# Mixing weights, first matrices and first read back on ScalarE's queue, and two late tiles behind the first forward transforms

## What is computed

```python
X = np.fft.rfft(x, axis=1)
Yr = Xr @ w_r - Xi @ w_i + b_r
Yi = Xr @ w_i + Xi @ w_r + b_i
Y = soft_threshold(Yr, 0.01) + 1j * soft_threshold(Yi, 0.01)
y = np.fft.irfft(Y, n=3008, axis=1)            # (6016, 256) as tokens
h = y @ moe_w_in                                # 256 -> 2048
g = maximum(h, 0) + alpha * minimum(h, 0)
z = g @ moe_w_out                               # 2048 -> 256
h2 = z @ moe2_w_in
g2 = where(h2 >= 1, h2, where(h2 <= -1, 0, (h2 + 1) ** 2 / 4))
out = g2 @ moe2_w_out
```

## Time and profile before

| | us |
|---|---|
| median of 3 runs | 1197.14 |
| lowest and highest | 1196.10, 1198.14 |
| the profiled execution | 1194.89 |
| its span | 1193.1 |
| TensorE busy | 1173.4 (98%) |
| VectorE busy | 886.8 (74%) |
| ScalarE busy | 850.2 (71%) |
| GpSimd busy | 691.8 (58%) |

### The profile page before, as it was taken

The page is one execution under the profiler, slowest core; times in us unless marked ns, Lnnn a source line. Parts: engine busy times, 40 slices in busy tenths (PEclk is TensorE's granted clock), DMA queues, the critical chain, the costliest instruction groups (busy, mean ns, idle before and its releaser), DMA issues.

```text
span 1193.1 us, 21060 instructions
## 1 busy us (share of the span) xinstructions
PE 1173.4 (98%) x6948; PEld 1135.1 (95%) x6948; DVE 886.8 (74%) x1686; ACT 850.2 (71%) x1874; POOL 691.8 (58%) x724
## 2 busy tenths in 40 slices
PE   8999999999999999999999999999999999999997
PEld 3899889999999999999999999999999999999997
DVE  4777677777777777777778787778778787878765
ACT  2335557777777777777767788888878787878775
POOL 3006546666575766766556566665657575757553
PEclk9999999999999999999999999999999999999999
DMA  9777620211112101212005500101010101010001
GB/s 307 247 251 238 189 66 1 94 40 54 41 49 72 67 27 41 85 37 67 19 1 177 190 23 2 26 1 27 1 27 1 27 1 24 4 19 9 13 15 27
DMA packets 64125, 77.75 MB, mean 65 GB/s; under 512 B 31216, under 2 KB 43632, under 8 KB 64016
## 3 DMA queue, kind: packets, MB, share of 16 engines
q1 hardware_dynamic: 60532, 69.92, 19.0%
q10 hardware_dynamic: 3484, 6.48, 1.6%
HBM read 46.10 MB, written 30.28 MB: 64 GB/s over the span
## 4 chain that ended last, share of the span: by engine, by line
PE 93%; POOL 3%; ACT 1%; DVE 1%; issue 1%; DMA 1%; SPq 0%; POOLq 0%; DVEq 0%; ACTq 0%
PE bank L1153 80%; PE bank L1120 6%; PE bank L1139 2%; PE bank L1094 2%; PE bank L1130 2%; PE bank L1105 2%; POOL g_lo L515 2%; DMA x_sb<-x 1%; POOL prep_raw L541 0%; POOL xc_lo L490 0%; PE bank L1078 0%; ACT g_hi L762 0%; ACT prep_hi L785 0%; SPq L325 0%; DVE y_sum L856 0%
## 5 line engine op out<-in xcount | busy, mean ns | idle before, releaser
L515 POOL TENSOR_TENSOR g_lo<-g_sb,g_hi 128x376 fp32r<-128x376 f32 x510 | 505.1, 1001 | 374.2 <-ACT g_hi L762 373.7
L1153 PE MATMUL bank<-g_hi,w_out_hi 128*128 128x376 f32 x1024 | 345.1, 337 | 0.9 <-POOL g_lo L515 0.4
L1153 PE MATMUL bank<-g_lo,w_out_hi 128*128 128x376 f32 x1024 | 342.0, 334 | 0.0
L1153 PE MATMUL bank<-g_hi,w_out_lo 128*128 128x376 f32 x1024 | 341.8, 334 | 0.0
L1153 PE MATMUL bank<-xc_hi,w_in_hi 128*128 128x376 f32 x896 | 302.3, 337 | 0.6 <-DVE partial L921 0.2
L1153 PE MATMUL bank<-xc_hi,w_in_lo 128*128 128x376 f32 x896 | 300.4, 335 | 0.0
L1153 PE MATMUL bank<-xc_lo,w_in_hi 128*128 128x376 f32 x896 | 298.5, 333 | 0.0
L762 ACT ACTIVATE g_hi<-g_sb 128x376 fp32r<-128x376 f32 x512 | 261.0, 510 | 44.1 <-DVE g_sb L958 28.5
L1153 PEld LDWEIGHTS bank<-g_hi,w_out_hi 128*128 128x128 f32 x1024 | 192.3, 188 | 8.8 <-POOL g_lo L515 7.6
L1153 PEld LDWEIGHTS bank<-g_lo,w_out_hi 128*128 128x128 f32 x1024 | 192.4, 188 | 0.0
L1153 PEld LDWEIGHTS bank<-g_hi,w_out_lo 128*128 128x128 f32 x1024 | 192.3, 188 | 0.0
(11 more groups left out here) (82 smaller groups left out, 1534.3 us busy)
## 6 DMA issues: line engine op xcount, KB each, us to landing
gc<-group_consts SPq DMA_DIRECT2D x24, 256.0 KB, 4.3
zt<-slots_scratch SPq DMA_DIRECT2D x24, 256.0 KB, 4.2
inverse_scratch<-v_sb SPq DMA_DIRECT2D x24, 256.0 KB, 2.8
ut<-inverse_scratch SPq DMA_DIRECT2D x16, 384.0 KB, 4.8
slots_scratch<-a_sb ACTq DMA_DIRECT2D x15, 384.0 KB, 4.2
x_sb<-x SPq DMA_DIRECT2D x16, 256.0 KB, 4.0
prep_raw<-wpack SPq DMA_DIRECT2D x16, 256.0 KB, 2.6
out<-yt SPq DMA_DIRECT2D x120, 32.0 KB, 1.6
```

What stands on the lines that cost most here:

```text
L515: pool.tensor_tensor(g_lo[kind][:, :], g_sb[n % 3][:, :], g_hi[kind][:, :].bitcast(f32), ALU.subtract)\
L1153: done = pe.matmul(out_ap, w, g, start=first and n == 0, stop=last_one and n == 2, skip_group_check=unchecked)
```

## The change

- `FIRST_TILES` goes from 12 to 11. The late tiles are now 11 to 15, behind `forward` of the steps 0, 1, 4, 8 and 12. Tile 10 is loaded by SyncE with the early ones, ahead of the store of tile 7.
- `wm_raw` and `gc[0]` are issued by ScalarE, right behind its store of tile 7. `zt[0]` is issued by ScalarE behind its copy of tile 9 and a wait for the nine stores; `wm_hi` and, on VectorE, `wm_lo` follow there, ahead of the copies of tile 10.
- SyncE, behind the store of tile 7, issues the tiles 11 and 12 and the bias, and only then waits for the stores, for the pairs 1 and 2.
- `FULL_TILES` goes from 2 to 1: tile 1 is filled by VectorE, a fifth fill, and comes in two transfers.

```diff
-FIRST_TILES = TILES_PER_BATCH + 4
-LATE_TILES = {1: FIRST_TILES, 4: FIRST_TILES + 1, 8: FIRST_TILES + 2, 12: FIRST_TILES + 3}
-LATE_LOADS = {4: FIRST_TILES + 2, 6: FIRST_TILES + 3}
+FIRST_TILES = TILES_PER_BATCH + 3
+LATE_TILES = {0: FIRST_TILES, 1: FIRST_TILES + 1, 4: FIRST_TILES + 2, 8: FIRST_TILES + 3, 12: FIRST_TILES + 4}
+LATE_LOADS = {4: FIRST_TILES + 3, 6: FIRST_TILES + 4}
-FULL_TILES = 2
+FULL_TILES = 1
@@ SyncE
-            for t in range(1, TILES_PER_BATCH + 2):
+            for t in range(1, FIRST_TILES):
                 load_x(t)
             t = TILES_PER_BATCH - 1
             sp.wait_ge(a_right, t + 1)
             sp.dma_start(az_rows[0, 0:ROWS_PAD, t * TILE_COLS + HALF_COLS:(t + 1) * TILE_COLS],
                          a_tile(t)[:, HALF_COLS:]).then_inc(a_stored[0], 16)
-            load_x(TILES_PER_BATCH + 2)
-            load_x(TILES_PER_BATCH + 3)
-            load_matrices(0)
-            sp.wait_ge(a_stored[0], 16 * (TILES_PER_BATCH + 1))
-            load_values(0)
-            sp.dma_start(wm_raw[:, :], wmix).then_inc(wm_in, 16)
             load_x(FIRST_TILES)
+            load_x(FIRST_TILES + 1)
             sp.dma_start(bias_sb[:, :], bias).then_inc(bias_in, 16)
+            sp.wait_ge(a_stored[0], 16 * (TILES_PER_BATCH + 1))
             for p in range(1, SLOTS):
                 load_values(p)
                 load_matrices(p)
-            load_x(FIRST_TILES + 1)
+            load_x(FIRST_TILES + 2)
@@ ScalarE, in the loop over the first tiles
-            act.wait_ge(wm_in, 16)
-            act.activation(wm_hi[:, :], wm_raw[:, :], ACT.Copy).then_inc(wm_hi_ready, 1)
+                if t == TILES_PER_BATCH - 1:
+                    act.dma_start(wm_raw[:, :], wmix).then_inc(wm_in, 16)
+                    act.dma_start(gc[0][:, :], group_consts[0, :, :]).then_inc(gc_in[0], 16)
+                if t == TILES_PER_BATCH + 1:
+                    act.wait_ge(a_stored[0], 16 * (TILES_PER_BATCH + 1))
+                    act.dma_start(zt[0][:, :, :], az_pairs[0, :, :, :]).then_inc(zt_in[0], 16)
+                    act.wait_ge(wm_in, 16)
+                    act.activation(wm_hi[:, :], wm_raw[:, :], ACT.Copy).then_inc(wm_hi_ready, 1)
@@ VectorE, in the loop over the first tiles
-            dve.wait_ge(wm_hi_ready, 1)
-            dve.tensor_tensor(wm_lo[:, :], wm_raw[:, :], wm_hi[:, :].bitcast(f32), ALU.subtract)\
-               .then_inc(wm_lo_ready, 1)
+                if t == TILES_PER_BATCH + 1:
+                    dve.wait_ge(wm_hi_ready, 1)
+                    dve.tensor_tensor(wm_lo[:, :], wm_raw[:, :], wm_hi[:, :].bitcast(f32), ALU.subtract)\
+                       .then_inc(wm_lo_ready, 1)
```

More of the change, by code:

```diff
@@ L365, in _ @@
                          a_tile(t)[:, HALF_COLS:]).then_inc(a_stored[0], 16)
-            load_x(TILES_PER_BATCH + 2)
-            load_x(TILES_PER_BATCH + 3)
-            load_matrices(0)
+            load_x(FIRST_TILES)
+            load_x(FIRST_TILES + 1)
+            sp.dma_start(bias_sb[:, :], bias).then_inc(bias_in, 16)
             sp.wait_ge(a_stored[0], 16 * (TILES_PER_BATCH + 1))
-            load_values(0)
-            sp.dma_start(wm_raw[:, :], wmix).then_inc(wm_in, 16)
-            load_x(FIRST_TILES)
-            sp.dma_start(bias_sb[:, :], bias).then_inc(bias_in, 16)
             for p in range(1, SLOTS):
```

## The result

The changed kernel took 1204.31 us (median of 6 runs, 1200.22 to 1206.23), the kernel before 1197.14 on the same chip (6 runs, 1196.10 to 1198.16). The ratio is 1.0053, 95% interval 1.0039 to 1.0068: slower by about 6 to 7 us, where 3.5 was forecast. The median lies 0.7 us above the upper end of the stated range, 1203.6. The profiled execution took 1204.87 us with a span of 1203.1, 10.0 more than the span of before.

A forecast was written before the change was run, and what follows sets the result against it. TensorE, busy 98% of the span, was taken as the bound, so delay before mix(0) counts in full: +1.3 us (landing of zt[0]) + 2.2 (clock) = +3.5, 1198.4 profiled, 1200.6 us with the 2.25 median offset; range 1195.2 to 1203.6.

The forecast's parts named there:

- What bounds the kernel: Whole kernel: TensorE, busy 98% of the span; what happens before the first mixing product moves everything behind it one for one.
- The order on TensorE: From zt[0]'s landing to mix(0): forward(0), tile 11, forward(1), tile 12 take 4.3 us, against 4.24 before.
- Z: Time at which zt[0] has landed: 30.22 us before, forecast 31.5, ends 30.1 and 33.1; break-even 30.2.
- The landing of zt[0]: Read back ahead of mix(0): loaded queues bring it at 31.5 in place of 30.22, 1.3 us later.
- The stores lose what it takes: Queues in 20 to 22 us: tile 10's 0.39 MB takes bytes from the stores, less 0.13 MB tile 1 no longer carries.
- Tile 1 in two parts: Start of the kernel: tile 1 is down at about 6.5 us, cost nothing, at worst 1 us late.
- the queue argument of the prediction: From 22.2 us on, 1.45 MB up to zt[0] at 0.18 MB/us takes 8.1 us, plus 1.2: landing at 31.5.
- The copies behind the weights: Copies of tile 10 behind the weights' splitting, needed by tile 11: cost nothing, at most about 1 us.
- The clock: After 6.6 us idle behind tile 10, forward(0) and tile 11 run at 1.2 GHz: +2.2 us, bounds 0 and 2.6.
- A: Rival, start of the kernel: zt[0] meets a short queue, lands at 27.8, mix(0) at 32.1; 1194.8 us if clock holds; chance 0.17.
- B: Rival: landing 30.2 with fallen clock (+2.2) or 31.5 with held clock (+1.3); about 1198.9 us; chance 0.30.
- D: Rival: worse sharing, short rows of zt[0] and matrices lose turns; landing 33.1, clock 2.6, +5.5, 1202.6 us; chance 0.15.

The follow-up runs named there:

- e3: The changed kernel with five added products on zeros, results unused, ahead of forward(0); 1201.50 us, ratio 1.0028 to the kernel before.
- j2: The kernel before with only the order moved: tile 11 behind forward(0), wm_hi and wm_lo behind its copies; 1198.80 us, ratio 1.0006.
- j4: The kernel before with weights, first matrices and zt[0] issued by ScalarE, tiles 10 to 12 behind the last store, TensorE order kept; 1198.70 us, ratio 1.0008.
- h1: The kernel before with two added products, results unused, ahead of the fourth token product group; 1196.34 us, ratio 0.9988.
- f2: The changed kernel with tile 1 whole, tile 10 behind tile 7's store, weights and first matrices back on SyncE; ScalarE issues zt[0] alone; 1201.07 us, ratio 1.0025.
- j5: The kernel before with only zt[0] moved, issued by ScalarE behind its copy of tile 9 into an empty queue; 1198.35 us, ratio 1.0004.

## Why the prediction was right in direction and short in size

The forecast was +3.5 us, and it came out at +7.2 in the medians, beyond the upper end of the range (1203.6) by 0.7 us. The direction and the two mechanisms held; one term was mis-sized by 3 us.

- **What bounds the kernel.** Right. All of mix(0)'s delay reached the end; the first product of the layers is later by 9.84 us (167.13 against 157.29) and the end by 10.0.
- **The order on TensorE.** The path Z + 4.3 is right: 4.32 us in e3 at the full clock. That the order in itself costs nothing holds only with Z fixed and the clock held; the profile of j2 shows the cover that it takes away.
- **The landing of zt[0], forecast +1.3, measured +4.35.** This is the term that failed. "The stores lose what it takes" (tile 10) was right as to bytes (0.42 MB in place of 0.74 in 20 to 22), but the step that failed is the issue of zt[0]. The working let it leave near 25 and had the bytes ahead of it in its queue decide; it left at 29.12, because the last store landed that late. I moved only bytes, not instructions: tile 10's two issues also stand ahead of the last store in SyncE's own queue, and they took 1.60 and 1.31 us in place of 0.6. The last store left at 22.56, after a copy done at 21.39, and landed at 29.1 where the working implied about 25. The issue of the last store at 20.48 was carried over from the trace of before unexamined, though that trace has slow issues where both queues are loaded:

```profile
14.27 1.38 SPq L326 DMA_DIRECT2D x_sb<-x  x1
```

  The instructions are the smaller part all the same (1.14 us, and 0.94 by the later copy); most is the store's own landing, 3.0 us slower in the loaded queues. e2, with tile 10 behind the store, has Z at 32.80.
- **Tile 1 in two parts, forecast nothing, at worst 1 us.** Failed as well: "the idle stretch behind tile 10 covers it too, unless it delays the stores" named the condition, and it was met. 0.66 MB fewer by 12 us, waits for the tiles 7 to 10, and 2.2 us at Z in the profile of e1. With tile 1 whole, e1 has Z = 32.37, 2.15 us later than before; in that kernel the queue argument of the prediction (31.5, at most 33.1) would have held.
- **The copies behind the weights.** Nothing, as said: wm_lo and tile 10's copies were done at 32.5, before Z.
- **The clock, forecast +2.2, measured +1.94** in the profile (1.86 by e3). Right, though the idle stretch was 4.74 us, not 6.6, since the tiles ahead of it were late too. That no gap in the trace of before is long enough to test the clock was wrong: its wait of 2.43 us ahead of the fourth token group is such a gap, and behind it the clock fell in nine of twelve profiles.
- **Behind mix(0), forecast nothing.** The profile shows 3.7 us there, which would count as a miss by the prediction's own test. The 0.66 us up to the first token group lies within what `ut` differs by from profile to profile, and the fall near 150 us is found in before as well, so neither is shown to be a cost of the change. The profile-to-median offset of 2.25 us that the prediction added has, by the table above, much to do with this fall.
- **The rivals.** A needed Z below 30.2 and is out. B needs one of its terms missing; both were there. D had the right signs, "the sharing is worse", with Z = 33.1; the measured Z lies 1.5 us beyond it, and by another cause than the short rows that it named.

## What to carry to other kernels

When a transfer is moved ahead of another in one engine's queue, count its issue instructions under load as well as its bytes: of the 2.1 us by which the store behind it left later 1.1 were such instructions, and it landed 3 us more slowly. A transfer that "costs nothing" at the start may still starve the queues there, so look at the bytes moved by the time of the first contention, not only at who waits for the tile. And before two profiled spans are subtracted, see whether the clock fell in one of them at a wait that both have: here that was 2.9 of 10.0 us. One profile of each kernel also hides how far landings scatter: with the same transfers zt[0] left between 27.5 and 30.4.

## What the runs showed of the hardware that was not expected

- The granted clock fell after idle stretches of 1.70, 2.01, 2.11, 2.43 and 2.58 us, up to about 2 us after work had begun again, and in other executions it held after 2.22 and 2.43 us. The fall lasted 3 to 7 us and cost 1.4 to 2.9 us. The Trainium skill, TensorE: Matmul & The Clock Gate, section "Why this matters for your kernels", asks to leave no long idle gaps between bursts; the traces agree that gaps before work lower the clock, and here gaps of about 2 us were at times enough.
- DMA issue instructions on SyncE and ScalarE, 0.31 to 0.6 us as a rule, took up to 2.4 us each while both queues were loaded (1.99 for one part of tile 9, 2.05 for `gc` in j4, 2.38 for one part of tile 8 in h1). The wait stands in the engine's order, so it delays the copies behind it: ScalarE's copy of tile 8 started at 23.07, right behind the issues of the weights (1.35 us) and the matrices.
- An empty second queue gave a read with 1 KB rows 20 and 22% of the bytes beside larger packets in the other (2.9 KB in the mean in f2, 2.7 in j5), and the read took 8.4 and 6.1 us against 5.8 in the full queue.
